# Second expert product with its weights stationary, its result kept transposed in SBUF; group width one of eight; feature weights split late

## What is computed

```python
f = 1.0 / (1.0 + np.exp(-f_logit))
for t in range(S):
    state = f[:, :, t, :, None] * state + np.einsum('bhd,bhe->bhde', k[:, :, t], v[:, :, t])
    y[:, :, t] = np.einsum('bhd,bhde->bhe', q[:, :, t], state)   # state: 48 x 48 per head
# x = y, tokens as rows. 8 experts, one for each token
expert_idx = argmax(xn @ en.T / tau);  gate_w = softmax(...)[expert_idx]
for e in range(8):
    h = np.maximum(x[mask] @ w1[e], 0.0)          # 384 -> 1024
    out[mask] = gate_w[mask, None] * (h @ w2[e])  # 1024 -> 384
# last stage, all tokens
a = x @ w_a;  b = x @ w_b                         # 384 -> 1536, twice
return (a * b) @ w_out                            # 1536 -> 384
```

## Time and profile before

| | |
|---|---|
| median of 3 runs | 918.28 us (917.61 to 923.69) |
| the profiled execution | 918.64 us, its span 917.4 us |
| PE busy | 875.3 us, 95% of the span |
| DVE, ACT, POOL busy | 366.3, 325.3, 115.6 us |
| granted clock over the span | 0.98 |

### The profile page before, as it was taken

One profiled execution on the slowest core, in us unless ns is written; L12 is line 12 of the kernel. 1 busy time (PEld: TensorE's weight loads), 2 busy tenths in 40 slices (PEclk: granted clock), 3 DMA queues, 4 the chain that ended last, 5 costly groups with the idle time before them and its releaser, 6 DMA issues.

```text
span 917.4 us, 14464 instructions
## 1 busy us (share of the span) xinstructions
PE 875.3 (95%) x5213; PEld 800.6 (87%) x5214; DVE 366.3 (40%) x623; ACT 325.3 (35%) x622; POOL 115.6 (13%) x152
## 2 busy tenths in 40 slices
PE   5999999938999999998899999999999999999996
PEld 5999999928999989997888888888888888888885
DVE  5666666586554543464132232232132222223222
ACT  6555555414554444453322222122122122122221
POOL 2121111121111101136000010010010001001001
PEclk9999999958999999999999999999999999999999
DMA  9665555136655444543100020020010002000000
GB/s 230 187 168 173 163 154 180 53 106 174 206 166 180 141 133 144 186 128 128 67 3 1 1 70 1 1 69 0 0 59 10 0 0 69 0 0 35 0 1 35
DMA packets 41823, 78.41 MB, mean 85 GB/s; under 512 B 11775, under 2 KB 31292, under 8 KB 40764
## 3 DMA queue, kind: packets, MB, share of 16 engines
q1 hardware_dynamic: 25916, 51.19, 19.1%
q10 hardware_dynamic: 11520, 15.73, 4.8%
q0 software_dynamic: 4352, 11.03, 3.9%
HBM read 62.18 MB, written 15.76 MB: 85 GB/s over the span
## 4 chain that ended last, share of the span: by engine, by line
PE 94%; DVE 2%; issue 1%; ACT 1%; DMA 1%; POOL 1%; SPq 0%; DVEq 0%; ACTq 0%
PE bank L965 32%; PE bank L983 16%; PE bank L887 13%; PE bank L899 12%; PE bank L806 4%; PE bank L772 3%; PE bank L745 3%; PE bank L809 2%; PE bank L802 2%; PE bank L821 2%; PE bank L780 1%; PE bank L875 1%; PE bank L761 1%; PE bank L952 1%; DMA xin<-xd,token 1%
## 5 line engine op out<-in xcount | busy, mean ns | idle before, releaser
L965 PE MATMUL bank<-x_hi,wab_hi 128*128 128x512 f32 x432 | 168.1, 389 | 2.5 <-DVE x_lo L1280 2.5
L965 PE MATMUL bank<-x_hi,wab_lo 128*128 128x512 f32 x432 | 169.4, 392 | 0.0
L965 PE MATMUL bank<-x_lo,wab_hi 128*128 128x512 f32 x432 | 169.2, 392 | 0.0
L1286 DVE TENSOR_TENSOR h<-bank,a_sb 128x512 f32<-128x512 f32 x72 | 49.9, 693 | 275.2 <-ACT a_sb L702 275.2
L702 ACT ACTIVATE a_sb<-bank 128x512 f32<-128x512 f32 x72 | 43.1, 599 | 281.4 <-PE bank L965 281.3
L983 PE MATMUL bank<-wout_hi,h_hi 128*128 128x384 f32 x288 | 97.5, 338 | 0.7 <-DVE h_lo L1290 0.7
L983 PE MATMUL bank<-wout_hi,h_lo 128*128 128x384 f32 x288 | 97.1, 337 | 0.0
L965 PEld LDWEIGHTS bank<-x_hi,wab_hi 128*128 128x128 f32 x432 | 81.1, 188 | 18.2 <-DVE x_lo L1280 2.8
L983 PE MATMUL bank<-wout_lo,h_hi 128*128 128x384 f32 x288 | 96.7, 336 | 0.0
L965 PEld LDWEIGHTS bank<-x_hi,wab_lo 128*128 128x128 f32 x432 | 81.1, 188 | 17.0
L965 PEld LDWEIGHTS bank<-x_lo,wab_hi 128*128 128x128 f32 x432 | 81.1, 188 | 15.7
(11 more groups left out here) (184 smaller groups left out, 1419.3 us busy)
## 6 DMA issues: line engine op xcount, KB each, us to landing
w_raw<-in_w SPq DMA_DIRECT2D x8, 1536.0 KB, 6.9
w_raw<-in_w SPq DMA_DIRECT2D x32, 384.0 KB, 3.7
qk_all<-in_chan SPq DMA_DIRECT2D x48, 192.0 KB, 3.3
ys<-y_sb ACTq DMA_DIRECT2D x32, 192.0 KB, 2.5
tok<-in_tok SPq DMA_DIRECT2D x24, 192.0 KB, 3.7
wab_raw<-in_wab SPq DMA_DIRECT2D x24, 192.0 KB, 3.7
tok<-in_tok ACTq DMA_DIRECT2D x24, 192.0 KB, 3.5
xd<-xst ACTq DMA_DIRECT2D x24, 192.0 KB, 3.5
```

Source lines behind the costliest of these rows:

```text
L965: last_op = pe.matmul(bank[2 * i + m][:, :], w[:, KM * m + k, cols], x[:, k, :], start=(k == 0 and w is wab_hi and x is x2_hi), stop=(k == ...
L1286: dve.tensor_tensor(h2[i][:, :], bank[2 * i + 1][:, :], a_sb[i][:, :], ALU.mult).then_inc(h_ready, 1)
```

## The change

- TensorE's second expert product `down(j, m)` now holds a block of `w2` (128 hidden by 128 output columns) stationary and moves the group's `n` tokens, 3 blocks `m` of 24 matmuls. The result is transposed already: 128 output values by `n` tokens.
- `n` is one of eight widths, 352 to 448 by 16, and 512. VectorE counts for each group how many of the first seven are below its number of tokens (`tile_width`). TensorE picks one of eight copies of the whole group (`tile`) by nested `If`s (`narrow`), the wider half of the copies standing first. There are eight copies for group 0, eight in the loop and eight for the last group; the loop now runs over `range(1, FULL - 1)`, groups 1 to 6, with no test, and one further copy of width 512 in a loop of its own is skipped here.
- ScalarE copies each `m` into `yT` in SBUF, [128, 3, 3584] fp32 (`keep_y`), in place of four copies and four stores to `ys`. The last stage reads its tokens from `yT`; the loads from `ys` and all transposes of it are gone. `x2_hi` has two buffers, and its low part is written over `yT`.
- The feature weights are loaded during attention as before, whole, without a wait; they are split by block `f` (768 columns at once) in the last group and the first step of the last stage, `wout` too, by blocks of 384 columns.
- The last stage is written out for all six steps. `features(u + 1, 0)` stands ahead of the last `project` of step `u`, and `results` behind the first block of the next step. VectorE clears three more strips of PSUM at the start.

```diff
+    AHEAD = KM + 2
+    WIDTHS = [*range(352, 449, 16), T]
+    NW = len(WIDTHS)
...
-    wab_hi = sb("wab_hi", [P, C, F2], fp32r)
-    wab_lo = sb("wab_lo", [P, C, F2], fp32r)
+    wab_raw = sb("wab_raw", [P, C, F2])
+    wab_lo = sb("wab_lo", [P, C, F2], fp32r, at=cursor[0] - 4 * C * F2)
+    yT_at = cursor[0]
+    yT = sb("yT", [P, KM, TOKENS + T])
+    yT_lo = sb("yT_lo", [P, KM, TOKENS + T], fp32r, at=yT_at)
...
+        for b in range(B):
+            load_wab(0, b)
...
-                sp_eng.wait_ge(wab_lo_ready, before + 1)
...
-        def load_y(u):
-            sp_eng.dma_start(yg[:, :, :], ys_steps[:, bass.ds(u, 1), :, :].rearrange("p u b d -> p (u b) d")).then_inc(y_loaded, 16)
...
+        transposed = sp_eng.snap(used * TB)
...
+        sp_eng.wait_ge(x1T_done, transposed)
+        sp_eng.dma_start(wout_raw[:, 0:FK, :].rearrange("p k n -> p (k n)"), wout_in[:, 0:FK * DM]).then_inc(wout_loaded[0], 16)
+        sp_eng.wait_ge(w2l, split)
+        sp_eng.dma_start(wout_raw[:, FK:FB2, :].rearrange("p k n -> p (k n)"), wout_in[:, FK * DM:FB2 * DM]).then_inc(wout_loaded[1], 16)
...
-                    act.wait_ge(wab_loaded[b], c * 16 + 16)
-                    act.activation(wab_hi[:, bass.ds(c, 1), DM * b:DM * b + DM].rearrange("p c n -> p (c n)"),
-                                   wab_raw[:, DM * b:DM * b + DM], ACT.Copy).then_inc(wab_hi_ready, 1)
...
-        def store_y(j, t, begin, first=False):
-            act.wait_ge(down_done[t], j + 1)
+        def keep_y(j, m, begin, first=False):
+            act.wait_ge(down_done, j * KM + m + 1)
             if not first:
-                act.wait_ge(ys_written[t], j * 16)
-            act.activation(y_sb[:, t, :], bank[4 + t][:, 0:DM], ACT.Copy).then_inc(y_copied, 1)
-            act.wait_ge(y_copied, j * TB + t + 1)
-            if not first and t == 0:
-                for earlier in range(1, TB):
-                    act.wait_ge(ys_written[earlier], j * 16)
-            act.dma_start(ys[bass.ds(begin + t * P, P), :], y_sb[:, t, :]).then_inc(ys_written[t], 16)
+                act.wait_ge(y_copied, j * KM + m)
+            act.activation(yT[:, m, bass.ds(begin, T)], bank[4 + m][:, :], ACT.Copy).then_inc(y_copied, 1)
+
+        def wab_high(f):
+            cols = slice(P * f, P * f + P)
+            act.activation(wab_hi[:, :, cols], wab_raw[:, :, cols], ACT.Copy).then_inc(wabh, 1)
+
+        def wout_high(f):
+            act.wait_ge(wout_loaded[f >= FK], 16)
+            act.activation(wout_hi[:, f, :], wout_raw[:, f, :], ACT.Copy).then_inc(wouth, 1)
+
+        def x2_high(u, i, k):
+            act.activation(x2_hi[i][:, k, :], yT[:, k, u * U:u * U + U], ACT.Copy).then_inc(x2h, 1)
...
+                keep_y(j, 0, begin, first)
...
+                for m in range(1, KM):
+                    keep_y(j, m, begin, first)
+            else:
+                act.wait_ge(wab_loaded, TILES * 16)
+                wab_high(0)
+                for m in range(KM):
+                    wab_high(m + 1)
+                    keep_y(j, m, begin)
+                    act.wait_ge(y_copied, j * KM + m + 1)
+                    x2_high(0, 0, m)
...
+                if f == 0 and not first:
+                    results(u - 1, u == 1)
+                if first and f + 2 < FB2:
+                    wout_high(f + 2)
+                if first and f + AHEAD < FB2:
+                    wab_high(f + AHEAD)
+                if not last and 3 <= f < 3 + KM:
+                    x2_high(u + 1, (u + 1) % 2, f - 3)
...
+        def down(j, m, n, paced):
+            cols = slice(P * m, P * m + P)
...
+                for w, h in ((w2_hi, h1_hi), (w2_hi, h1_lo), (w2_lo, h1_hi)):
+                    last_op = pe.matmul(bank[4 + m][:, 0:n], w[:, f, cols], h[:, f, 0:n],
+                                        start=(f == 0 and w is w2_hi and h is h1_hi), stop=(f == FB1 - 1 and w is w2_lo))
+            last_op.then_inc(down_done, 1)
+
+        def tile(j, n, first, last):
+            up(j, n)
...
+            for m in range(KM):
+                down(j, m, n, m == 0)
+                if m == 0 and not last:
+                    transpose_x(j + 1)
+
+        def group(j, first=False, last=False):
+            chosen = pe.value_load(tile_width[0:1, bass.ds(j, 1)], min_val=0, max_val=NW - 1)
+            pe.wait_ge(x1l, j * TB + TB)
+
+            def narrow(low, high):
+                if high - low == 1:
+                    tile(j, WIDTHS[low], first, last)
+                    return
+                middle = (low + high) // 2
+                with pe.If(chosen > middle - 1):
+                    narrow(middle, high)
+                with pe.If(chosen < middle):
+                    narrow(low, middle)
+
+            narrow(0, NW)
...
-        used = pe.value_load(tiles_used[0:1, 0:1], min_val=FULL, max_val=NT)
         final = pe.value_load(tiles_used[0:1, 1:2], min_val=FULL - 1, max_val=NT - 1)
         group(0, first=True)
-        with pe.Fori(1, NT - 1) as j:
-            with pe.If(j < final):
-                group(j)
+        with pe.Fori(1, FULL - 1) as j:
+            group(j)
+        with pe.If(final > FULL - 1):
+            with pe.Fori(FULL - 1, NT - 1) as j:
+                with pe.If(j < final):
+                    pe.wait_ge(x1l, j * TB + TB)
+                    tile(j, T, False, False)
         group(final, last=True)
...
-        def transpose_y(u, k):
...
+            if f == 0:
+                order = [(m, k) for m in range(2) for k in range(KM - 1)] + [(m, KM - 1) for m in range(2)]
...
+        features(0, 0)
+        for u in range(C):
+            for f in range(1, FB2):
                 features(u, f)
-                if f:
-                    project(u, f - 1, first=first)
-            if not last:
-                for k in range(KM):
-                    transpose_y(u + 1, k)
-            project(u, FB2 - 1, first=first)
-
-        step(0, first=True)
-        with pe.Fori(1, C - 1) as u:
-            step(u)
-        step(C - 1, last=True)
+                project(u, f - 1)
+            if u + 1 < C:
+                features(u + 1, 0)
+            project(u, FB2 - 1)
...
+        for m in range(KM):
+            dve.memset(bank[4 + m][:, DM:], 0.0)
...
-                    dve.wait_ge(wab_hi_ready, c * B + b + 1)
-                    dve.tensor_tensor(wab_lo[:, bass.ds(c, 1), cols], wab_raw[:, cols].rearrange("p (c n) -> p c n", c=1),
-                                      wab_hi[:, bass.ds(c, 1), cols].bitcast(fp32), ALU.subtract).then_inc(wab_lo_ready, 1)
...
+        by_width = [P, NT, NW - 1]
+        link(dve.tensor_tensor(r["p2"][:, :, :], over(col(r["left"][:, :]), by_width), over(row(width[:, :]), by_width), ALU.is_gt))
         link(dve.tensor_reduce(r["parts"][:, :], r["p2"][:, :, :], AX.X, ALU.add))
...
+        def wab_low(f):
+            cols = slice(P * f, P * f + P)
+            dve.wait_ge(wabh, f + 1)
+            dve.tensor_tensor(wab_lo[:, :, cols], wab_raw[:, :, cols], wab_hi[:, :, cols].bitcast(fp32), ALU.subtract).then_inc(wabl, 1)
+
+        def wout_low(f):
+            dve.wait_ge(wouth, f + 1)
+            dve.tensor_tensor(wout_lo[:, f, :], wout_raw[:, f, :], wout_hi[:, f, :].bitcast(fp32), ALU.subtract).then_inc(woutl, 1)
+
+        def x2_low(u, k):
+            cols = slice(u * U, u * U + U)
+            dve.wait_ge(x2h, u * KM + k + 1)
+            dve.tensor_tensor(yT_lo[:, k, cols], yT[:, k, cols], x2_hi[u % 2][:, k, :].bitcast(fp32), ALU.subtract).then_inc(x2l, 1)
...
+                wab_low(0)
+                for k in range(KM):
+                    wab_low(k + 1)
+                    x2_low(0, k)
```

More of the change, by code:

```diff
@@ L133, in attention_moe_ffn @@
     qT = [sb(f"qT{b}", [P, HP, P]) for b in range(B)]
-    kT = [sb(f"kT{b}", [P, HP, P]) for b in range(B)]
     masked_at = cursor[0]
@@ L141, in attention_moe_ffn @@
     ssq = sb("ssq", [P, B])
[L142 to L143 removed]
+    kT = [sb(f"kT{b}", [P, HP, P]) for b in range(B)]
     assert cursor[0] <= w1_lo_at + 4 * KM * F1, cursor[0]
@@ L917, in group @@
[L917 to L934 removed]
+                pe.wait_ge(y_copied, j * KM)
@@ L1307, in _ @@
         dve.wait_ge(row_ready, 2)
-        results(0, first=True)
-        with dve.Fori(1, C - 1) as u:
+        for u in range(1, C):
             step(u)
-            x2_low(u + 1)
-            results(u)
-        step(C - 1)
         results(C - 1)
```

243 lines of the change are left out of this document (75 added, 168 removed).

## The result

| | before | forecast | after |
|---|---|---|---|
| median | 918.93 us (917.61 to 923.69) | 909 us (881 to 940) | 962.86 us (958.38 to 967.19) |
| ratio, 95% interval | | 0.99 | 1.047 (1.040 to 1.053) |
| span of the profiled execution | 917.4 us | 908.1 us | 965.9 us |
| TensorE's start of group 0 | 210.33 us | 214.7 us | 216.15 us |
| first to last matmul of the groups | 241.5 us | | 291.1 us |

The account below looks back on a forecast made before the run. TensorE, busy 95% of the span, was taken as the bound. Savings of 21.4, 7.9, 4.7, 2.4 and 0.4 us took 917.4 to 880.6; late code added 27.5 and span-to-median 0.9, giving 909 us, range 881 to 940.

Parts of the forecast that it names:

- Widths: Expert groups' matmuls: both products take 72 matmuls of the group's own width, 352 to 432 columns, saving 21.4 us together.
- Transposes, loop, hand-over, start: Last stage, group loop and first chunk: savings of 7.9, 4.7, 2.4 and 0.4 us respectively.
- The empty turns: TensorE's loop rounds for absent groups, before the last group: removing them saves 2.84 idle plus 1.87 clock, 4.7 us.
- the cover at the hand-over: Groups to last stage: 12 matmuls (2.7 us) hide a 2.0 us copy and split; 2.4 us gained, 0 if it fails.
- Work moved late: Feature-weight splits in the last group and first step of the last stage: hidden under TensorE's matmuls, no cost.
- The sum without code: Whole kernel, all savings taken from the 917.4 us span before any cost of fetching instructions: 880.6 us.
- The code of TensorE: TensorE's jumps over skipped group copies wait for instruction blocks: 21.9 us of stalls plus 5.6 of clock, 27.5 us.
- Groups 2, 3, 5, 6: Boundaries into these groups: code blocks seen before or next in line, so 0 us of stalls if they stay.
- I take 2.7: Each TensorE jump to a late block: 2.7 us, from SyncE's only long jump; stated bounds nothing to 2.7 and more.
- the slower rival: Group loop drives out its own code, two late blocks or so at each of five boundaries: 936 us, chance 0.27.
- The way out: TensorE leaving the last group: one late block, about covered by the sequencer running ahead of the matmuls.
- Clock, 1.87 us a stall, three stalls: TensorE's lowered clock after each of three stalls within the group stream: 1.87 us each, 5.6 us.

## Why the prediction was wrong

**Widths: right.** Without the low clock the groups' matmuls cost 203.5 us (twice the second products' 101.76), forecast 202.6 (224.0 before, less 21.4; the 204.6 in the expectations is my slip); `up` of 400 columns, the only one with no idle ahead, takes 12.96 us, forecast 12.95.

**Transposes, loop, hand-over, start: right.** The last stage is 6.3 us shorter, forecast 5 x 1.31 = 6.6, the sixth lies in the last group. The empty turns were worth 4.3 us alone, forecast 4.7. With one width the last stage begins without idle, so the cover at the hand-over holds. With 384 and 512 the four terms together are 15.7 us, forecast 15.4; with the idle and the wide groups' gain named there set aside, they are some 16.5.

**Work moved late: right.** No idle of TensorE is put down to a split of the feature weights; the only idle at L937 is 1.8 us of issue.

**The sum without code: right.** 965.9 - 73.2 of issue - 12.7 of clock (14.9 in all `up`s, less the 2.2 that group 0 had before) = 880.0 us; forecast 880.6. (One sentence ahead of the prediction is wrong: `features` does 18 matmuls of 512 columns a block, not 36. No price hung on it, since the 6.2 us of a block came from the chain. In the prediction, the parts of a boundary without late code add up to 2.4 us, not 2.65; that is 0.25 us a boundary, and no verdict hangs on it.)

**The code of TensorE: the step that failed.** Forecast 27.5 us, measured 85.9 in the profiled execution (73.2 of idle, 12.7 of clock). The forecast took a block once fetched as kept for good; the runs show loops of jumps whose blocks are gone again when they are needed. By its own terms:

- *"Groups 2, 3, 5, 6: blocks seen before or next in line, 0 if they stay."* They did not stay. The boundaries to groups 2, 5 and 6 had 3, 4 and 2 late jumps, 38.9 us. This is the larger part. At the places where I counted late blocks the count was exact for group 0 (2), 0 to 1 (3) and group 4 (2), and one too many for the last group.
- *"I take 2.7, SyncE's being the only row of a long jump."* A jump over a block or more costs TensorE 3.3 us at the least in quiet, 4.7 behind another and up to 7.5 beside the weight loads; the 18 late ones of the changed kernel take 2.7 to 7.5, 4.6 in the mean. At the places forecast the stalls are 32.5 us in place of 21.9. I had written "2.7 us and more" as the bound and then used 2.7 at both ends of the range, in the slower rival too. An upper end was missing.
- *The way out, "about covered by the lead"*: 1.8 us.
- *Clock, 1.87 us a stall, three stalls*: 12.7 us, six stalls at 1.7 to 2.5 us; the term was right for one and short in number.

10.6 + 1.8 + 38.9 + 7.1 = 58.4 us, the whole of 85.9 - 27.5.

**The chances.** The slower rival named the right mechanism and the right sign, at 0.27. Its 936 us is 27 us short of the median, since it took two late blocks a boundary at 2.7 us. (From 36.8 us of stalls and clock on the kernel is slower than before; that is 1.4 such boundaries beyond the forecast, not two.) Its evidence, 10.5 blocks against loops of three, was all that the trace had on the question, and nothing in it spoke for a store as large as ten. The loops of straight code now put the limit at seven blocks, and it is lower with jumps: loops of 3.9 and 4.9 blocks were late again in later rounds. The sentence that I set beside the sum was the better guide: the Trainium skill, in "Runtime: NRT & Kernel Launch", section "Instruction fetch mechanics", gives TensorE's instruction memory as 128 KiB or eight blocks, and by it the new loop does not fit. The runs agree with that figure (7 blocks kept, 8 not). The same section says that a taken branch out of the current two-page window must wait for its page; with that the runs do not agree as it stands, since jumps over 3, 6 and 10 blocks took 0.2 us once their targets had been brought in.

## What to carry to other kernels

Count the code of a hardware loop in blocks of 250 instructions before multiplying copies of its body. On TensorE a few copies keep most of the gain: two widths chosen for the data gave 3.2% here, and 384 with 512, which leaves nothing out, 1.7%, where eight lost 4.7%; even a copy that is never run cost a branch of 5.3 us, and 7.7 us of the kernel's time, where it had to be jumped over at an exposed place. A loop of jumps below eight blocks is no promise: of the loops with several copies only those of two were free of late branches in every round. And where the only row of a cost is that of another engine in another stretch, it is one value and no upper end: the range must allow for its being longer and coming more often.

## What the runs showed of the hardware

- TensorE holds about eight blocks of 16 KB of straight code. Loops of 7 are transferred once; a loop of 8 moves 10 blocks every round and takes 33.8 us a round, where the loop of 7 takes 23.3.
- A jump past the next block that is not held takes 3.3 to 4.0 us in quiet, for 1 block as for 8, and 4.1 to 4.9 us right behind another late one. It brings two blocks.
- With jumps less is kept, and not by size alone: a loop of 3.9 blocks was late at the same jump in two successive visits, one of 4.9 was late in every round, one of 5.2 only in its first, and one of 11 blocks with a single jump over 10 only in its first.
- A late jump is longer beside data: the same jump took 4.98 us at a DMA share of 0.18 and 7.47 at 0.56.
- TensorE can stand still behind a jump that was not late itself: 1.15 us in the middle of `up`, 13 matmuls in.
- After 4.25 us of idle TensorE's clock stood at 1.2 GHz, and the following 512-column `up` took 3.0 us more.
